# Three edits to a recurrence-and-experts kernel: logs of two chunks at once, a new order of the products in groups with turns, one weight part computed earlier

## The reference

```
for t in range(S):
    m_new = max(f[t] + m, i[t])
    C = exp(f[t] + m - m_new) * C + exp(i[t] - m_new) * outer(v[t], k[t])
    n = exp(f[t] + m - m_new) * n + exp(i[t] - m_new) * k[t]
    y[t] = sigmoid(o[t]) * (C @ q[t]) / max(abs(n @ q[t]), 1)
for e in range(4):
    out += p[:, e] * (relu(x @ w1[e]) @ w2[e])
y = ((out @ w_a) * (out @ w_b)) @ w_out
```

## Time and profile before

| | |
|---|---|
| median of 3 runs | 618.39 us (618.35 to 618.46) |
| the profiled execution | 618.21 us, of which its span is 616.1 us |
| TensorE (PE) busy | 603.9 us, 98% |
| VectorE (DVE), ScalarE (ACT), POOL busy | 356.5, 291.3, 178.3 us |
| mean granted TensorE clock | 0.994 of full |

### The profile page before, as it was taken

The page is one execution under the profiler, slowest core; times in us unless marked ns, Lnnn a source line. Parts: engine busy times, 40 slices in busy tenths (PEclk is TensorE's granted clock), DMA queues, the critical chain, the costliest instruction groups (busy, mean ns, idle before and its releaser), DMA issues. The chain is left out here.

```text
span 616.1 us, 10977 instructions
## 1 busy us (share of the span) xinstructions
PE 603.9 (98%) x4011; PEld 584.5 (95%) x4011; DVE 356.5 (58%) x705; ACT 291.3 (47%) x618; POOL 178.3 (29%) x246
## 2 busy tenths in 40 slices
PE   8999999999999999999999999999969999999997
PEld 7888999999999999999999999998869999999997
DVE  6667974454463534553436344696746665666555
ACT  4778735333443344433444435746624443444332
POOL 3566430024420152301252003413114530453000
PEclk9999999999999999999999999999979999999999
DMA  4765542002321022320214000230001420120011
GB/s 126 205 216 184 156 125 61 0 1 68 96 63 37 1 46 47 110 61 1 46 23 113 29 12 1 57 96 29 29 11 27 120 62 12 31 61 0 1 65 64
DMA packets 21092, 38.39 MB, mean 62 GB/s; under 512 B 3552, under 2 KB 11344, under 8 KB 21040
## 3 DMA queue, kind: packets, MB, share of 16 engines
q1 hardware_dynamic: 19104, 35.03, 20.3%
q10 hardware_dynamic: 1936, 2.67, 1.4%
HBM read 26.42 MB, written 1.97 MB: 46 GB/s over the span
## 5 line engine op out<-in xcount | busy, mean ns | idle before, releaser
L1626 PE MATMUL PS<-w2h,hh 128*128 128x320 f32 x528 | 165.3, 313 | 4.9 <-DVE w2l L1013 4.8
L1626 PE MATMUL PS<-w2l,hh 128*128 128x320 f32 x528 | 163.9, 310 | 0.0
L1626 PE MATMUL PS<-w2h,hl 128*128 128x320 f32 x528 | 163.7, 310 | 0.0
L1545 PE MATMUL PS<-xop,wop 128*128 128x384 f32 x400 | 139.4, 349 | 0.4
L1548 PE MATMUL PS<-xop,wop 96*128 96x384 f32 x400 | 135.3, 338 | 0.0
L1546 PE MATMUL PS<-xop,wop 128*128 128x384 f32 x400 | 135.3, 338 | 0.0
L1547 PE MATMUL PS<-xop,wop 128*128 128x384 f32 x400 | 135.1, 338 | 0.0
L715 ACT ACTIVATE hh<-c_s 128x384 fp32r<-128x384 f32 x120 | 62.9, 524 | 101.9 <-DVE c_s L1201 29.0
L1626 PEld LDWEIGHTS PS<-w2h,hh 128*128 128x128 f32 x528 | 99.9, 189 | 5.7 <-issue 5.1
L1626 PEld LDWEIGHTS PS<-w2l,hh 128*128 128x128 f32 x528 | 100.0, 189 | 0.0
L1626 PEld LDWEIGHTS PS<-w2h,hl 128*128 128x128 f32 x528 | 99.7, 189 | 0.0
(11 more groups left out here) (148 smaller groups left out, 812.3 us busy)
## 6 DMA issues: line engine op xcount, KB each, us to landing
s<-in_wt SPq DMA_DIRECT2D x24, 256.0 KB, 3.3
kvo<-in_tok SPq DMA_DIRECT2D x12, 480.0 KB, 4.0
wop<-t1h SPq DMA_DIRECT2D x48, 112.0 KB, 2.2
qk<-in_qk_t SPq DMA_DIRECT2D x24, 160.0 KB
s<-in_w SPq DMA_DIRECT2D x12, 320.0 KB, 3.1
wop<-t1l SPq DMA_DIRECT2D x24, 112.0 KB, 2.2
s<-in_w_out SPq DMA_DIRECT2D x12, 160.0 KB, 2.2
out_y<-acc SPq DMA_DIRECT2D x12, 160.0 KB, 1.9
```

What stands on the lines that cost most here:

```text
L1545: nc.tensor.matmul(to, ws[0], xs[0], start=opens, stop=False, skip_group_check=True)
L1626: got = nc.tensor.matmul(bank, left, (w2l if part == 1 else w2h)[p][:, f, :], start=opens and part == 0, stop=closes and part == 2)
```

## The change

**Logs.** The gates of chunks 0 and 1 (`EARLY = 256` columns) are loaded first and their logs made together on 16 partitions; `lf0` now lies in a tile that is free at that time. The scan of the other columns, and with it `m_ready`, comes after them. The rows of chunk 1 come from these tiles, not from `rest_logs`, and `dec_l` of chunk 1 is written by VectorE, so that `load_dec_l(1)` falls away. SP loads q and k of unit 1 before the first high rows. ScalarE issues the low rows before its part of `m_r`. VectorE does `weigh(0)` before `rest_logs`. `keep_busy(9)` becomes `keep_busy(4)`.

**Order in groups with turns** (29, 30, 33, 34). The products come as 0, 2, 1, 4, 5, 3, 6; the turns stand behind products 0, 4 and 5, where before they stood behind 0, 2 and 2. The chunks, and the lists of ScalarE and VectorE in these groups, are written anew as `turning_expert` and `turning_gated`.

**One low weight part.** `low_w2(19)` was issued in group 36, ahead of `make_c22`; now it is issued in group 35, between `make_ab1` and `make_c12`.

TensorE's order, turns and chunks (the second tuple is for `n > FIRST`), and the filling at the start:

```diff
+        ORDER = (0, 2, 1, 4, 5, 3, 6)
...
+            return range(7) if turning(n) is None else ORDER
...
+        def done(n, i):
+
+            return made(n, list(order(n)).index(i) + 1)
...
-            return {0: (0,), 2: (1, 2)}.get(i, ())
+            return {0: (0,), 4: (1,), 5: (2,)}.get(i, ())
...
-                return (3, 6, 1, 0, 6, 6, 1, 6, 4, 3) if n <= FIRST else (0, 5, 0, 0, 4, 5, 0, 4, 0, 0)
+                return (3, 6, 0, 1, 2, 5, 1, 6, 6, 6) if n <= FIRST else (0, 2, 0, 1, 1, 2, 0, 6, 6, 0)
...
-            keep_busy(9)
+            keep_busy(4)
...
-                for i in range(4 if n < PLAIN else 7):
+                for i in order(n):
```

SP's list:

```diff
+            sp.wait_ge(qk_zero, 2)
+            load_qk(1)
+            load_first_high_row(0)
+            load_first_high_row(1)
             sp.wait_ge(m_ready, 1)
             sp.dma_start(m_r[:, 1, :], m[:, P + 1:S + 1]).then_inc(m_in, 16)
-            load_first_high_row(0)
-            load_first_high_row(1)
-            sp.wait_ge(qk_zero, 2)
-            load_qk(1)
             load_kvo(1)
-            load_dec_l(1)
             load_rows(2)
             load_rows(3)
-            sp.wait_ge(dec_l_in[1], 32)
```

ScalarE's new lists (`b1`, `b2` are the set whose first or second group of turns this is):

```diff
+            def turning_expert(n):
+
+                b1, b2 = set_at(n, 1), set_at(n, 2)
+                keep_p1(n)
+                keep_turn(n, 0)
+                replicate_late(b1, 2)
+                replicate_late(b2, 5)
+                keep_u2(n)
+                if b2 is not None:
+                    x_high(b2, 0)
+                high_c11(n)
+                keep_w(n)
+                keep_turn(n, 1)
+                replicate_late(b1, 3)
+                if b2 is not None:
+                    x_high(b2, 1)
+                high_c21(n)
+                keep_turn(n, 2)
+                if b2 is not None:
+                    x_high(b2, 2)
+                prepare_weights(n)
+                high_c22(n)
+                prepare_sums(n)
+                high_c12(n)
+                replicate_late(b1, 4)
...
+            def turning_gated(n):
+
+                b1, b2 = set_at(n, 1), set_at(n, 2)
+                keep_p1(n)
+                keep_turn(n, 0)
+                high_product(n - 1, 1)
+                keep_u2(n)
+                replicate_late(b1, 2)
+                replicate_late(b2, 5)
+                keep_w(n)
+                keep_turn(n, 1)
+                prepare_early(n)
+                replicate_late(b1, 3)
+                keep_turn(n, 2)
+                high_product(n, 0)
+                if b1 is not None:
+                    x_high(b1, 0)
+                    x_high(b1, 1)
+                if b2 is not None:
+                    x_high(b2, 2)
+                    x_high(b2, 3)
+                prepare_weights(n)
+                replicate_late(b1, 4)
```

VectorE: the logs, the moved low part, and its new gated list:

```diff
             first_logs()
             for u in range(NU):
+                weigh(u)
                 if u == 0:
                     rest_logs()
-                weigh(u)
-                if u == 0:
                     rest_ends()
...
-                if n == FIRST + 4:
-                    w2_lows(n - 2)
...
+                if b3 is not None:
+                    w2_lows(n - 1)
                 make_c12(n)
...
+            def turning_gated(n):
+
+                b1, b2 = set_at(n, 1), set_at(n, 2)
+                if b1 is not None:
+                    add_tiles(n, range(HB, UB))
+                make_c11(n)
+                low_product(n - 1, 1, c12_s[:, :])
+                w2_lows(n - 1)
+                make_ab1(n)
+                if b2 is not None:
+                    x_sum(b2, 0)
+                make_c22(n)
+                if b1 is not None:
+                    x_low(b1, 0)
+                if b2 is not None:
+                    x_low(b2, 2)
+                make_c12(n)
+                low_product(n, 0, c11_s[:, :])
+                make_ab2(n)
+                if b1 is not None:
+                    x_low(b1, 1)
```

More of the change, by code:

```diff
@@ L886, in expert_group @@
             def expert_group(n):
-                b0, b1, b2, b3, b4 = (set_at(n, k) for k in range(5))
+                b0, b3 = set_at(n, 0), set_at(n, 3)
                 keep_p1(n)
[L890 to L896, removed]
                 high_c11(n)
@@ L1096, in logs_of @@
                     dve.wait_ge(done, n + 4)
-                rows = lf.shape[0]
-                nc.vector.tensor_tensor_scan(lsum, ones[0:rows, :], lf, 0.0, ALU.mult, ALU.add).then_inc(done, 1)
+                rows, cols = lf.shape
+                for at in range(0, cols, P):
+                    nc.vector.tensor_tensor_scan(lsum[:, at:at + P], ones[0:rows, :], lf[:, at:at + P], 0.0, ALU.mult, ALU.add).then_inc(done, 1)
+                n += cols // P - 1
                 dve.wait_ge(done, n + 5)
@@ L1299, in expert_group @@
                 p = n % NP1
-                b2, b3 = (set_at(n, k) for k in (2, 3))
+                b3 = set_at(n, 3)
                 if p == 1:
@@ L1308, in expert_group @@
                     late_low(1)
-                if b2 is not None:
-                    x_low(b2, 0)
-                    x_low(b2, 1)
                 if b3 is not None:
@@ L1324, in expert_group, with turning_expert @@
                 make_c12(n)
+                if b3 is not None:
+                    x_sum(b3, 3)
+                else:
+                    w2_lows(n)
+                low_relu(n, 3, c12_s[:, :])
+                if b3 is not None:
+                    w2_lows(n)
+            def turning_expert(n):
+                b2 = set_at(n, 2)
+                if n % NP1 == 1:
+                    add_tiles(n, range(HB, UB))
+                make_c11(n)
+                low_relu(n, 0, c11_s[:, :])
+                if b2 is not None:
+                    x_low(b2, 0)
+                    x_low(b2, 1)
+                low_relu(n, 1, PS[:, A_BANK, 0:HT])
+                make_c22(n)
+                low_relu(n, 2, c22_s[:, :])
+                make_c12(n)
                 if b2 is not None:
                     x_low(b2, 2)
[L1327 to L1330 removed]
                 low_relu(n, 3, c12_s[:, :])
[L1332 to L1333 removed]
+                w2_lows(n)
             def gated_group(n):
                 p = n % NP1
[L1338 to L1340 removed]
+                b3, b4 = set_at(n, 3), set_at(n, 4)
                 make_c11(n)
@@ L1347, in gated_group @@
                     low_product(n - 1, 1, c12_s[:, :])
-                if p == 1 and n > FIRST + 1:
+                if p == 1:
                     add_tiles(n, range(HB, UB))
-                if b1 is not None:
-                    w2_lows(n - 1)
-                    x_low(b1, 0)
-                if b2 is not None:
-                    w2_lows(n - 1)
-                    x_sum(b2, 0)
-                    x_low(b2, 2)
                 if b3 is not None:
```

131 lines of the change are left out of this document (62 added, 69 removed).

## The result

The changed kernel takes 610.64 us (median of 6 runs, 610.04 to 630.18) against 618.42 for the kernel before on the same chip (6 runs, 618.20 to 624.48): ratio 0.985, 95% interval 0.981 to 0.989. (Both sets hold a few disturbed runs; the ratio leaves them out.) The profiled execution took 610.64 with a span of 608.5, against 618.21 and 616.1: 7.6 us less in the trace, 7.8 in the medians. Forecast were 10.3 us and 608.1. The range (605.8 to 611.0) held, but 610.64 lies only 0.4 us inside its upper end. A quarter of the gain is missing, and the question is where.

A forecast was written before the change was run, and what follows sets the result against it. TensorE, busy 98% of the span, was taken as the bound. Gains of 7.2 + 1.0 + 1.6 + 0.5 = 10.3 us from the profiled 618.21 gave 607.9, or 608.1 as median; range 605.8 to 611.0.

The forecast's parts named there:

- main mechanism: Group 36: moving low_w2(19) earlier removes TensorE's wait for w2l and the half clock behind it; 7.2 us gained.
- The moved low part: low_w2(19) moved behind make_ab1 of group 35: product 5 of group 36 at 453.95 instead of 461.14; gain 7.2 us, bounds 6.2 to 7.7.
- it costs nothing there: Group 35, VectorE: the moved part needs 0.49 of the 0.73 us in which VectorE waits for TensorE before make_c12.
- The start: First units: products(1) at 13.0 instead of 14.02, log_weights(0) at 10.2; gain 1.0 us, bounds 1.8 gain to 0.8 loss.
- `turn_rest_logs` would not wait for VectorE: Start: a slack near 0.8 us hides the later rest_logs and rest_ends; a wait there would show the prediction wrong.
- Groups 29 to 31: New order: fewer waits for raw, but about 0.2 us for POOL's sums in groups 30 and 31; gain 0.5, bounds 1.0 and -0.5.
- the 1.2 of the walk: Groups 29 and 30: ScalarE's wait in prepare_sums for POOL's sums, put near 1.2 us, most of it hidden.
- Groups 33 to 35: New order of turns: of 3.4 us of pauses, 1.6 gained; bounds 3.2 and -0.5.
- the walk had 0.7: Group 33: product 3 waits for ScalarE's copy of turn 2, a pause of 0.7 us.
- the terms are smaller: Rival: the reordering gains nothing, as the copies of turn 2 come behind prepare_early; 610.2 us, chance 0.13.
- The rows' late arrival: Rival at the start: rows land late behind q and k; 609.1 us, or 609.9 at the late bound; chance 0.13.
- The clock fell at the start: Rival: the clock falls at the start because five fillings went; 610.8 us, chance 0.03.

The follow-up runs named there:

- narrow_sum: Changed kernel with POOL's last subtractions for x narrowed from 384 to 128 columns, leaving out part of that sum: 610.57 us, ratio 0.986.
- logs_only: Kernel before with only the new start (logs of two chunks, SP's and ScalarE's lists, 4 fillings): 617.39 us, ratio 0.997.
- two_fixes: Changed kernel with prepare_weights earlier in groups 29 and 30, and dec_l and rows of chunk 2 issued ahead of unit 3's q and k: 610.28 us.
- order_only: Kernel before with only the new order of products, turns, chunks and lists: 617.33 us, ratio 0.998.
- weights_early: Changed kernel with prepare_weights in groups 29 and 30 ahead of the second high part of x and high_c21: 610.67 us, ratio 0.988.
- turn_copy_first: Changed kernel with prepare_early behind the third turn's copy on ScalarE in groups 33 and 34: 611.67 us, ratio 0.990.
- filled_pause: Kernel before with 13 unread matmuls of 128 columns put into TensorE's pause in group 36: 616.94 us, ratio 0.998.
- rows_first: Changed kernel with dec_l and rows of chunk 2 issued on SP ahead of unit 3's q and k and the probabilities: 611.27 us, ratio 0.989.
- three_fixes: Changed kernel with the edits of weights_early, rows_first and turn_copy_first together: 610.02 us, ratio 0.987.
- moved_only: Kernel before with only the low weight part moved to group 35: 611.82 us, ratio 0.988.
- qk_behind: two_fixes with q and k of unit 1 issued behind the two high rows on SP: 613.75 us, ratio 0.990.
- nine_fillings: two_fixes with keep_busy(9) instead of keep_busy(4): 610.03 us, ratio 0.987.

## Why the prediction was right, and where its sum was off

Its main mechanism held: one low part held the largest gain, the clock stayed full until TensorE's last matmul, and behind 80 us TensorE waits nowhere for over 0.6 us. The other three terms did not hold as well: together they were forecast at 3.1 us and brought 0.95 (0.14 - 0.53 + 1.34). That the time still fell within the range is owed to the size of the first term, and the profiled start was a lucky one: its `log_weights(0)` at 9.86 is the earliest of the eight profiles that have this start up to that step (9.86 to 11.01). What was off is the size of four terms, by 2.45 us in sum (0.3 + 0.86 + 1.03 + 0.26); with the 0.3 lost behind group 36 that makes the 2.7 between 10.3 and 7.6.

- **The moved low part: 7.2 forecast, 6.9 measured.** The term that was mis-sized is "it costs nothing there". The prediction looked for cover on VectorE alone. POOL's subtraction runs over the same stretch, and the low part took 1.20 us, so `make_c12` began 0.49 us later behind the start of group 35 (8.12 against 7.63). `narrow_sum` shows that it was POOL: with POOL done in time, the distance of products 5 is 8.17, what the prediction's own 453.95 - 445.78 makes. The Trainium skill's page "SBUF — State Buffer", section "SBUF: two separate sides", states that a VectorE operation with two inputs in SBUF and a GpSimd operation that reads SBUF exclude each other for a whole instruction. The trace agrees: the low part, which reads two SBUF tiles, ends 0.35 us behind the end of POOL's work (446.26 + 1.20 against 447.11), and takes 0.48 in `narrow_sum`, where POOL is done before it begins.
- **The start: 1.0 forecast, 0.14 measured.** The first step came out better than forecast: `log_weights(0)` at 9.86 (10.2), `products(1)` at 12.64 (13.0), with no wait for a DMA, 0.14 us behind the end of `weigh(0)` (11.82 + 0.68 = 12.50). The step that failed is the one that ended the walk at `turn_rest_logs`, ahead of `products(2)`, and counted `products(1)`'s lead as the end's. The next thing late was the `dec_l` of chunk 2, whose row `alo_r` was ready no earlier than `rest_logs` (12.41 to 16.0) allows, and was sent behind q and k of unit 3. `logs_only` shows the same `log_weights(4)` at 24.12 from a `products(1)` at 13.01; `two_fixes` moves it to 23.05, and with it `products(3)` comes 1.02 us earlier than before. So the forecast 1.0 is there to be had, with SP's order changed as well. The prediction's sign that `turn_rest_logs` would not wait for VectorE came out against it, by 0.35 us of weight load. The term behind that is `rest_logs`, taken over at 2.5 us: it took 3.6 (12.41 to 16.02), of which 1.1 is in the two steps shown above that run beside POOL (0.81 and 0.85 us against 0.28 and 0.29 before). It is the same oversight as for the moved low part, but no run takes POOL away here, so that its share is argued from the durations and not shown by an edit.
- **Groups 29 to 31: 0.5 forecast, -0.53 measured**, just past the lower bound of -0.5. The prediction named the mechanism (POOL's sums late, ScalarE held in `prepare_sums` with `high_c12` and `keep_p1` behind it) and took 0.2 for each of groups 30 and 31. In group 31 it is 0.86. `order_only` shows it without the other parts, and `weights_early` takes it away, at 0.2 in group 29. The wait of ScalarE was 3.15 us and not the 1.2 of the walk. In part POOL was slower: a subtraction of 128 columns takes 0.46 with VectorE idle (L524) and 0.66 at 398.94, while VectorE worked at L1019.
- **Groups 33 to 35: 1.6 forecast, 1.34 measured.** Groups 33 and 34 take 19.31 (19.2 forecast). The six pieces ahead of product 3 of group 33 and its pause took 1.40 instead of 6 x 0.148 = 0.89, 0.51 more, where the walk had 0.7. `turn_copy_first` shows that ScalarE's queue is its cause, and that the weights behind it are needed by the next group: the cure costs more than it brings.
- **Groups 37 to the end: 0 forecast, -0.3 measured.** This is not the change's doing. From the first matmul of group 37 to TensorE's last one ends, all 14 profiles fall into two sets, whatever the edit: 149.1 to 149.2 us (the kernel before, `order_only`, `filled_pause`, `weights_early`, `rows_first`, `turn_copy_first`, `three_fixes`, `narrow_sum`) and 149.4 (the changed kernel, `moved_only`, `logs_only`, `two_fixes`, `qk_behind`, `nine_fillings`). The profile of the kernel before happens to be of the first set and that of the changed kernel of the second. What parts the sets is open.

Of the rivals, the first ("the terms are smaller", 610.2) came half true: the new order brought 0.81 us (0.33 - 0.86 + 1.34) of the 2.1 forecast, and 610.64 is nearer to that rival than to the forecast. The rows' late arrival did not come true in the changed kernel's profile (9.86), but it did in others: `rows_first` 11.01, `weights_early` 10.63, `narrow_sum` 10.72, each behind a wait of 0.9 to 1.5 us for `llo`. The prediction's argument against it, that q and k should be mostly through by 7.4, was wrong: the records of their semaphore have them complete at 9.51 in the changed kernel, after the rows were issued. The clock fell at the start in the last two of these, which the prediction gave 0.03; `products(3)` came about 1.0 us later there (25.91 and 25.96 against 24.96). But falls are not owed to the five fillings that went: with the old start, too, the clock fell in two of four profiles (`moved_only` and `filled_pause`), behind waits of 1.3 and 1.2 us for `alo_r`, and it lasted 6.8 us.

## What to carry to other kernels

When an instruction is moved into a gap of its engine, look at what POOL does over the same stretch: in this kernel a gap of VectorE beside a running POOL operation was no cover for an operation with two SBUF inputs. When a step at the start is made earlier, walk on until the next transfer that depends on data computed later, and see what stands ahead of it on its queue; a lead at the first unit is worth nothing if a later one waits. Count a wait of an in-order engine with everything queued behind it, one group further than seems needed.

## What the runs showed of the hardware

- **The pace of the first matmuls varies from run to run.** The 28 records of filling that begin at 2.08 or 2.09 last until the first `products(0)` at 6.78 (`moved_only`) to 8.36 (`filled_pause`), with a granted clock of 1.00 in the view of stretches throughout. That is 0.17 to 0.22 us a record, where the later fillings take 0.13 (15 in 1.94 us in `moved_only`); what makes the first ones slower, and by how much, no run shows. So two profiled runs can differ by 1.6 us before `products(0)`. That is why small terms are read here from distances between milestones, and not from spans.
- **The lower clock lasted 3.4 or 6.8 us at a single pause**, and 13.7 us in the start of `qk_behind`. In group 36 it lasted 6.8 us in the kernel before and 3.4 in `order_only`, whose group took 14.34 instead of 15.33.
- **A late small transfer can cost more than its wait.** In the profiled run of `moved_only` `log_weights(4)` waited 1.29 us for `alo_r`, the clock was at its lower level for 6.8 us from 25.4 on, and `products(4)` came at 35.47 instead of 30.85: 4.6 us. `filled_pause` shows the same (a wait of 1.2, `products(4)` at 35.45); its profiled execution took 620.36. The length of the wait alone does not decide it: the 1.02 us of the changed kernel at this place, and 1.3 us for q and k ahead of `products(1)` in `moved_only`, had no fall. TensorE's timeline in `moved_only`, and the stretch behind it:

```profile
25.64 0.58 PE L1433 MATMUL PS<-mask,identb 128*128 128x512 bf16 x1 [1.29 <-DMA dec_l<-alo_r]
```

```profile
26.00:32.00 6.00, 6.00 (x32) 4.67 (x31) 2.03 (x4) 1.59 (x4) 1.30 (x2) 0.50 0.67 209
```
